# Gates and low parts in PSUM banks, GpSimd in pieces of 512 columns, the rounding of w_out on ScalarE: one change to a kernel of attention and two dense layers

## The chip, the cores and the metric

One core of a Trainium2 chip runs the whole program. The metric is the device time in microseconds. Of the kernel before there are three runs, median 811.41 us, from 811.0 to 811.67.

The engines are named as in the profile: PE is TensorE (PEld its weight load), DVE VectorE, ACT ScalarE, POOL GpSimd, SP SyncE, which issues nearly all loads and stores.

## The reference

```python
# attention: 2 x 8 heads, 768 tokens, 64 wide; mask: equal 6-bit sign buckets of q @ proj and k @ proj
scores = where(mask, (q @ k.T) / 8, -1e9)
attn = softmax(scores)            # sum + 1e-9
x = (attn @ v)                    # laid out as 1536 tokens x 512
# layer 1: 512 -> 2048 -> 512
h = x @ w_in;  g = where(h > 0, h, exp(min(h, 0)) - 1);  x = g @ w_out
# layer 2: 512 -> 2048 -> 512, its own weights
h = x @ w_in;  g = s * max(h, 0) ** 2 + b;  out = g @ w_out
```

All data are float32.

## The kernel before

Each float32 operand of a matrix product is held as two parts, "hi" (rounded to the short form that TensorE multiplies at full rate) and "lo" (the value less hi), and each product is three: hi x hi, hi x lo, lo x hi. Making hi is called rounding, making lo splitting.

**Attention.** Eight pairs of heads run one after the other, 12 units of 128 query rows to a pair. In each pair GpSimd splits q, k, v and every third transposed block (`split_third`), adds and scales the outputs into `x32` (`sum_x`, `scale_x`), and has slots for preparing the layers (`first_parts(i, half)`, two in a pair): it combines, rounds and splits the first weights, the first two blocks of w_out (`weights_out(0, 0)` and `(0, 1)`, the second in the slot (4, 0)) and the first chunk of x. SyncE asks for the second w_out block in pair 4 as well.

**The layers.** Each layer works on three chunks of 512 tokens (`CHUNKS`; q counts chunks through both layers, 0 to 5) and, for a chunk, in 8 steps of 256 hidden features (p = 0 to 7): 24 steps a layer (`LAYER`), 48 in all. A step has three parts.

1. `hidden(step)`, TensorE: the 512-deep product for 256 features x 512 tokens is done with seven block products instead of eight (`PRODUCTS`), from sums and differences of the blocks of w and x. Seven products of 6 matmuls with 256 columns (42 matmuls) go to four PSUM banks `h_ps[0..3]`, in the order of banks 0, 1, 2, 3, 0, 1, 3. Product 5 (bank 0 again) waits for ScalarE's copy of product 1 to `p1_sb` (shown as p_sb), product 6 (bank 1) for VectorE's sum U2, product 7 (bank 3) for U3. Products 1 to 4 wait for the sums C11, C12, C22, C21 of the step before.
2. The gate. VectorE makes the seven sums U2, U4, U3, C22, C11, C12, C21 (`sums`), each of one bank and one SBUF tile; the C sums are the hidden values, in `h_sb[0]` and `h_sb[1]`. For each half f ScalarE makes relu(-h) and exp(-that) (second layer: relu(h) and its square) in `r_sb[f]`; VectorE makes the gate in place in `h_sb[f]` (lines 1276 and 1278); ScalarE rounds it to `g_hi` (line 978 is the helper `copy` for all its copies); VectorE makes `g_lo` (line 1283). All of these are in SBUF.
3. `output(step)`, TensorE: 24 matmuls of 512 columns into the four banks `acc`, summed over the 8 steps of a chunk.

TensorE's order is hidden(step), output(step - 1), hidden(step + 1), and so on, so gates have the time of an output to be made. Its order at the start is: products 1 to 4 of hidden(0), the last pair's last P.V products, products 5 to 7, hidden(1), output(0).

VectorE's queue for a step: the sums, two gates, two low parts, `combine_w(step + 2)` (four additions of 256 columns, both operands in SBUF, which make the weight blocks' sums `wi_sum`), at p = 2 and 3 two operations each of `combine_x` for the next chunk, and in the second layer at p = 0 `keep_out`, the copy of the four `acc` banks to SBUF. ScalarE's: p_sb, `round_w(step + 1)` (three copies, the last of 1024 columns), relu and exp of both halves, two g_hi, at p = 0 in the first layer the copies of `acc` to `x32`, at p = 3 to 6 one `round_x`. GpSimd's: `weights(step + 1)`, the split of 512, 256 and 1024 columns (lines 590 and 593), then in 14 steps `weights_out` (step 0 to 5: the first layer's blocks 2 to 7; step 18 to 25: the second layer's blocks), a rounding (line 609) and a split (line 611) of 1024 columns each, then at p = 3 to 6 one `split_x` of 512 or 1024 columns. hidden(step) waits for `w_split`, at p = 0 for all four splits of x as well.

SyncE runs one queue in order: `load_w(step + 3)` waits for the split of step + 1, `load_wo` (line 385) for the split of the block before, as there is one buffer `wo_raw`; then stores.

Of the kernel before, what the change touches and what calls it, by code (L numbers as in the profile page):

```python
# [21 lines left out]
GROUPS = UNITS // HT  # L22
# [88 lines left out]
def build(nc, qk, v, planes_in, ident_in_d, w1_in, w1_out, w2_in, w2_out, s2, b2, out, inv_d):  # L111
    ctx = ExitStack()
    with ctx:
# [191 lines left out]
        out_kept = sem("out_kept")  # L305
        end_kept = sem("end_kept")
# [14 lines left out]
        def _(sp):  # L321
# [190 lines left out]
        def _(pool):  # L512
# [131 lines left out]
            def split_x(c, n):  # L644

                hi, lo = xb_hi[c % 2], xb_lo[c % 2]
                if n == B11:
                    x, dst = first_tokens(c % CHUNKS, lo)
                    return nc.gpsimd.tensor_tensor(dst, x, first_tokens(0, hi)[1].bitcast(F32), ALU.subtract)
# [3 lines left out]
                return nc.gpsimd.tensor_tensor(flat(lo[:, n:n + 2]), flat(xb_sum[c % 2][:, n:n + 2]),  # L653
                                               flat(hi[:, n:n + 2]).bitcast(F32), ALU.subtract)

            def first_parts(i, half):
# [14 lines left out]
                elif (i, half) == (4, 0):  # L671
                    weights_out(0, 1)
# [70 lines left out]
            for step in range(2 * LAYER):  # L743
# [11 lines left out]
                if q + 1 < 2 * CHUNKS and 3 <= p < 7:  # L755
                    n = p - 3
# [5 lines left out]
        def _(pe):  # L762
# [213 lines left out]
        def _(act):  # L976
# [95 lines left out]
            round_w(1)  # L1072
            for step in range(2 * LAYER):
# [4 lines left out]
                if 2 <= step + 1 < 2 * LAYER:  # L1078
                    round_w(step + 1)
                for f in range(2):  # L1080
                    act.wait_ge(added, SUMS * step + (C21 if f else C12))
                    wait(act, g_made, 2 * step - 1 + f)
                    nc.scalar.activation(r_sb[f][:], h_sb[f][:], ACT.Relu, scale=1.0 if layer else -1.0).then_inc(r_done, 1)  # L1083
                    act.wait_ge(r_done, 2 * step + f + 1)
                    nc.scalar.activation(r_sb[f][:], r_sb[f][:], ACT.Square if layer else ACT.Exp,  # L1085
                                         scale=1.0 if layer else -1.0).then_inc(e_done, 1)
                for f in range(2):
                    act.wait_ge(g_made, 2 * step + f + 1)
                    wait(act, g_free, 2 * step + f + 1 - GRING)
                    copy(g_hi[(2 * step + f) % GRING][:], h_sb[f][:]).then_inc(g_hi_done, 1)  # L1090
                if p == 0 and 0 < q <= CHUNKS:

                    for n in range(KT):
# [4 lines left out]
                        cols = slice(n * TOKENS + (q - 1) * CHUNK, n * TOKENS + q * CHUNK)  # L1098
                        copy(x32[:, cols], acc[n][:]).then_inc(y_kept, 1)
# [5 lines left out]
            act.wait_ge(out_kept, KT * CHUNKS)  # L1105
# [4 lines left out]
        def _(dve):  # L1110
# [105 lines left out]
            def combine_x(q, later):  # L1216

                c, n = q % CHUNKS, 4 * (q - 1)
                to = [as_x(xb_sum[q % 2][:, m]) for m in range(4)]
                b11, b12, b21, b22 = [x_of(c, d, t) for d in range(2) for t in range(2)]  # L1220
                if not later:
# [6 lines left out]
                    tt(to[T1], b12, b11, ALU.subtract).then_inc(xb_combined, 1)  # L1228
                    tt(to[T3], b22, b12, ALU.subtract).then_inc(xb_combined, 1)
                else:  # L1230
                    dve.wait_ge(xb_combined, n + 2)
                    tt(to[T2], b22, to[T1], ALU.subtract).then_inc(xb_combined, 1)
                    dve.wait_ge(xb_combined, n + 3)
                    tt(to[T4], b21, to[T2], ALU.subtract).then_inc(xb_combined, 1)

            def sums(step, part):
# [5 lines left out]
                for n in part:  # L1242
# [27 lines left out]
            def gate(step):  # L1270
                layer = step // LAYER
                for f in range(2):
                    h, e = h_sb[f][:], r_sb[f][:]
                    dve.wait_ge(e_done, 2 * step + f + 1)
                    if layer == 0:
# [71 lines left out]
```

## Time and profile before

| | us |
|---|---|
| median of three runs | 811.41 |
| the profiled execution | 812.05 |
| its span | 810.2 |
| PE busy | 755.5 |
| DVE busy | 667.2 |
| POOL busy | 523.0 |
| ACT busy | 490.6 |
| mean granted TensorE clock, share of full | 0.972 |

The profile is of one execution. The span runs from its first instruction to its last; the execution's own time is 1.85 us more. Busy time of an engine includes the time in which a started instruction is held back. Matmuls are pipelined and overlap in the records, so PE at 93% is not at its peak. The granted clock is the share of 2.4 GHz that TensorE was given; it has two levels, 1.00 and 0.50 (1.2 GHz), and slices of the page show a mean. A row with x2 merges two instructions of a kind. Square brackets hold the idle time of the engine before the instruction and what ended it.

### The profile page before, as it was taken

To read this page: it belongs to the slowest core of one execution; us is meant where nothing else is said; L and a number is where in the kernel's file an instruction comes from. 1 tells how busy PE (TensorE), PEld (TensorE's weight loads), DVE (VectorE), ACT (ScalarE), POOL (GpSimd) and SP (SyncE) were. 2 spreads that over 40 slices of the span, in tenths; PEclk is the share of its full clock that TensorE was granted. 3 is DMA by queue.
4 is the path that set the end of the run, shared out by engine and by line. 5 is a ranking of instruction groups with operands and counts; after the bars stand their busy time and mean duration, and the time that the engine had idled before them with its cause. 6 is when DMAs were issued, how large, how long until landed. Compare 5 with 4: busy or idle time off the path is not lost.

```text
span 810.2 us, 13830 instructions
## 1 busy us (share of the span) xinstructions
PE 755.5 (93%) x4617; PEld 684.1 (84%) x4617; DVE 667.2 (82%) x1191; ACT 490.6 (61%) x919; POOL 523.0 (65%) x370
## 2 busy tenths in 40 slices
PE   8999999799997887999989989698999999999998
PEld 6999999799986776998879878687887899798997
DVE  6888888688879888888888889888888878887774
ACT  8888887688854435565656454355556555565551
POOL 6688997999987777444654568775465444644440
PEclk9999999899998998999999989899999999999999
DMA  6576557456223221111111212212110311113101
GB/s 172 141 185 175 147 124 176 111 124 167 68 76 105 72 84 53 53 53 53 29 50 53 79 52 78 78 57 75 52 53 27 109 48 53 53 53 105 52 1 53
DMA packets 78286, 67.81 MB, mean 84 GB/s; under 512 B 9284, under 2 KB 66964, under 8 KB 78228
## 3 DMA queue, kind: packets, MB, share of 16 engines
q1 hardware_dynamic: 77940, 66.80, 30.2%
q8 instruction: 33, 0.54, 0.3%
q10 hardware_dynamic: 288, 0.26, 0.1%
q14 instruction: 25, 0.20, 0.1%
HBM read 46.23 MB, written 3.19 MB: 61 GB/s over the span
## 4 chain that ended last, share of the span: by engine, by line
PE 49%; DVE 32%; ACT 9%; issue 5%; POOL 4%; DMA 1%; SPq 0%; DVEq 0%; POOLq 0%; ACTq 0%
PE acc L886 14%; PE h_ps L866 14%; DVE g_lo L1283 8%; PE pt_ps L814 6%; DVE h_sb L1276 6%; ACT r_sb L1083 3%; PE pv_ps L829 3%; PE pv_ps L830 3%; PE s_ps L801 3%; PE s_ps L800 3%; DVE wi_sum L1212 3%; DVE h_sb L1278 3%; DVE wi_sum L1209 3%; ACT r_sb L1085 2%; DVE u_sb L1247 1%
## 5 line engine op out<-in xcount | busy, mean ns | idle before, releaser
L866 PE MATMUL h_ps<-xb_hi,wi_hi 128*128 128x256 f32 x672 | 198.6, 296 | 43.6 <-DVE u_sb L1247 36.8
L590 POOL TENSOR_TENSOR wi_lo<-w_raw,wi_hi 128x512 fp32r<-128x512 f32 x96 | 95.5, 1017 | 185.9 <-ACT wi_hi L978 185.9
L866 PE MATMUL h_ps<-xb_hi,wi_lo 128*128 128x256 f32 x672 | 193.4, 288 | 0.0
L866 PE MATMUL h_ps<-xb_lo,wi_hi 128*128 128x256 f32 x672 | 193.4, 288 | 0.0
L866 PEld LDWEIGHTS h_ps<-xb_hi,wi_hi 128*128 128x128 f32 x672 | 131.2, 195 | 53.3 <-DVE u_sb L1247 41.3
L866 PEld LDWEIGHTS h_ps<-xb_lo,wi_hi 128*128 128x128 f32 x672 | 131.8, 196 | 1.8
L866 PEld LDWEIGHTS h_ps<-xb_hi,wi_lo 128*128 128x128 f32 x672 | 131.9, 196 | 0.0
L593 POOL TENSOR_TENSOR wi_lo<-wi_sum,wi_hi 128x1024 fp32r<-128x1024 f32 x48 | 124.2, 2588 | 0.0
L1283 DVE TENSOR_TENSOR g_lo<-h_sb,g_hi 128x512 fp32r<-128x512 f32 x96 | 100.6, 1071 | 4.6 <-ACT g_hi L978 2.4
L1126 DVE TENSOR_SCALAR_CACHE_REDUCE probs<-s_ps 128x768 f32<-128x768 f32 x96 | 91.8, 957 | 11.1 <-PE s_ps L801 8.6
L978 ACT ACTIVATE g_hi<-h_sb 128x512 fp32r<-128x512 f32 x96 | 59.0, 626 | 67.4 <-DVE h_sb L1276 44.7
L886 PE MATMUL acc<-g_hi,wo_late 128*128 128x512 f32 x288 | 97.0, 409 | 0.0
L1276 DVE SCALAR_TENSOR_TENSOR h_sb<-r_sb,h_sb 128x512 f32<-128x512 f32 x48 | 79.3, 1666 | 21.2 <-ACT r_sb L1085 20.8
L978 ACT ACTIVATE wi_hi<-w_raw 128x512 fp32r<-128x512 f32 x94 | 44.0, 516 | 85.4 <-DVE wi_sum L1214 85.4
L886 PE MATMUL acc<-wo_late,g_hi 128*128 128x512 f32 x288 | 91.7, 390 | 0.0
L1083 ACT ACTIVATE r_sb<-h_sb 128x512 f32<-128x512 f32 x96 | 60.0, 625 | 52.0 <-DVE h_sb L1264 52.0
L984 ACT ACTIVATE probs<-probs,row_min 128x768 f32<-128x768 f32 x96 | 90.0, 937 | 2.1 <-DVE probs L1126 1.3
L814 PE MATMUL pt_ps<-ident_sb,probs 128*128 128x128 f32 x576 | 81.6, 278 | 5.8 <-ACT pt_raw L978 4.1
L814 PEld LDWEIGHTS pt_ps<-ident_sb,probs 128*128 128x128 f32 x576 | 69.1, 143 | 12.8 <-ACT pt_raw L978 4.4
L1278 DVE TENSOR_SCALAR h_sb<-r_sb,sb_scale 128x512 f32<-128x512 f32 x48 | 53.0, 1120 | 28.6 <-ACT r_sb L1085 28.6
L829 PE MATMUL pv_ps<-pt_hi,v_nat 128*128 128x384 f32 x192 | 72.8, 379 | 0.1
L886 PEld LDWEIGHTS acc<-g_hi,wo_late 128*128 128x128 f32 x288 | 58.2, 202 | 12.2
(116 smaller groups left out, 1747.7 us busy)
## 6 DMA issues: line engine op xcount, KB each, us to landing
w_raw<-w_in_dram SPq DMA_DIRECT2D x96, 256.0 KB, 3.1
wo_raw<-w_out_dram SPq DMA_DIRECT2D x32, 256.0 KB, 2.9
raw<-qk_dram SPq DMA_DIRECT2D x15, 384.0 KB, 5.4
qqk<-kt SPq DMA_DIRECT2D x15, 384.0 KB, 4.0
raw_v<-v_dram SPq DMA_DIRECT2D x16, 192.0 KB, 4.2
all_inv<-inv_dram SPq DMA_DIRECT2D x16, 192.0 KB
x_parts<-x_second SPq DMA_DIRECT2D x16, 192.0 KB, 5.4
qqk<-qqk SPq DMA_DIRECT2D x15, 192.0 KB, 2.7
```

The source lines that it names most:

```text
L590: nc.gpsimd.tensor_tensor(flat(lo[:, j]), loaded[:, cols], flat(hi[:, j]).bitcast(F32), ALU.subtract)
L593: return nc.gpsimd.tensor_tensor(flat(wi_lo[buf][:, S1:A11]), flat(wi_sum[buf][:]), flat(wi_hi[buf][:, S1:A11]).bitcast(F32), ALU.subtract)
L814: last = nc.tensor.transpose(pt_ps[n][:, r * P:(r + 1) * P], probs[k % SRING][:, (n * HT + r) * P:(n * HT + r + 1) * P], ident_sb[:])
L829: mm(pv_ps[:, 0:HALF], v_nat[par][:, kt, :], pt_hi[buf][:, kt, :], start=kt == 0, stop=False)
L866: last = mm(h_ps[bank][:, 0:Q], w[i][:, k * P:(k + 1) * P], x[j][:, k * Q:(k + 1) * Q], start=k == 0 and m == 0, stop=k == DK - 1 and m == 2)
L886: last = mm(acc[n][:], lhs, rhs, start=p == 0 and f == 0 and j == 0, stop=p == STEPS - 1 and f == 1 and j == 2)
L978: return nc.scalar.activation(dst, src, ACT.Copy)
L984: nc.scalar.activation(scores[:], scores[:], ACT.Exp, bias=row_min[:, k:k + 1], scale=-1.0, accum_out=row_sum[:, k, 0:1]).then_inc(exp_don ...
L1083: nc.scalar.activation(r_sb[f][:], h_sb[f][:], ACT.Relu, scale=1.0 if layer else -1.0).then_inc(r_done, 1)
L1126: ts(probs[k % SRING][:].rearrange("p (n c) -> p n c", n=2), s_ps[k % 2][:, :, 0:HALF], -SCALE, CEILING, ALU.mult, ALU.min, accum_out=row_ ...
L1276: last = nc.vector.scalar_tensor_tensor(h, e, 1.0, h, ALU.subtract, ALU.max)
L1283: tt(g_lo[n][:], h_sb[f][:], g_hi[n][:].bitcast(F32), ALU.subtract).then_inc(g_ready, 1)
```

## The change

- The exponential (the square) goes to bank `h_ps[f]`, the gate to bank `h_ps[2 + f]`; `g_hi` and `g_lo` are made from that bank. Products 1 and 2 of the next step wait for the two gates, products 3 and 4 for the two low parts, in place of the C sums.
- GpSimd's operations of 1024 columns on the weights' sums, on w_out's low part and on x are made in two of 512.
- ScalarE rounds w_out's blocks from the third on (`round_wo`, ahead of relu in its queue); GpSimd only splits them.
- In the attention, `weights_out(0, 1)` moves from the slot (4, 0) to (5, 0), and the combining and rounding of the first x move around it.
- hidden(0) is one piece ahead of the last P.V products; VectorE's `keep_x(PAIRS, -1)` moves behind all seven sums; ScalarE's `round_w(1)` moves behind the first p_sb.
- `combine_x` makes one difference a step at p = 1 to 4 instead of two at p = 2 and 3; `split_x` is at p = 4 to 7 instead of 3 to 6, behind weights and w_out.
- ScalarE copies `acc` of the first two chunks of the second layer too; VectorE copies the last chunk's (`keep_last`).

```diff
@@ SyncE, store(c)
-                        sp.wait_ge(out_kept, tile + 1)
+                        if c < CHUNKS - 1:
+                            sp.wait_ge(out_kept, tile + 1)
+                        else:
+                            sp.wait_ge(last_kept, m + 1)
@@ GpSimd
             def split_sums(buf):
-                return nc.gpsimd.tensor_tensor(flat(wi_lo[buf][:, S1:A11]), flat(wi_sum[buf][:]),
-                                               flat(wi_hi[buf][:, S1:A11]).bitcast(F32), ALU.subtract)
+                for j in (slice(S1, S3), slice(S3, A11)):
+                    last = nc.gpsimd.tensor_tensor(flat(wi_lo[buf][:, j]), flat(wi_sum[buf][:, j]),
+                                                   flat(wi_hi[buf][:, j]).bitcast(F32), ALU.subtract)
+                return last
...
                 pool.wait_ge(wo_landed, 32 * n + 32)
-                if layer:
-                    pool.wait_ge(g_free, 2 * (LAYER - STEPS + step) + 2)
-                nc.gpsimd.tensor_copy(wo(step, 0), wo_raw[:]).then_inc(wo_hi_done, 1)
+                if n < EARLY:
+                    nc.gpsimd.tensor_copy(wo(step, 0), wo_raw[:]).then_inc(wo_hi_done, 1)
                 pool.wait_ge(wo_hi_done, n + 1)
-                nc.gpsimd.tensor_tensor(wo(step, 1), wo_raw[:], wo(step, 0).bitcast(F32), ALU.subtract).then_inc(wo_split, 1)
+                for cols in (slice(0, DM), slice(DM, W)):
+                    last = nc.gpsimd.tensor_tensor(wo(step, 1)[:, cols], wo_raw[:, cols], wo(step, 0)[:, cols].bitcast(F32),
+                                                   ALU.subtract)
+                last.then_inc(wo_split, 1)
...
                 elif (i, half) == (4, 0):
+                    combine_x0(T1)
+                elif (i, half) == (4, 1):
+                    pool.wait_ge(x_scaled, PAIRS)
+                    combine_x0(T3, T2)
+                elif (i, half) == (5, 0):
                     weights_out(0, 1)
-                elif (i, half) == (4, 1):
-                    pool.wait_ge(x_scaled, PAIRS)
-                    combine_x0(T1, T3)
-                elif (i, half) == (5, 0):
-                    combine_x0(T2, T4)
                 elif (i, half) == (5, 1):
-                    round_x0(B11, B22)
+                    combine_x0(T4)
+                    round_x0(B11)
                 elif (i, half) == (6, 0):
+                    round_x0(B22)
                     round_x0(T1)
...
-                if step == 0:
-                    pool.wait_ge(pv_done, GROUPS * PAIRS)
...
-                if q + 1 < 2 * CHUNKS and 3 <= p < 7:
-                    n = p - 3
+                if q + 1 < 2 * CHUNKS and p >= 4:
+                    n = p - 4
@@ TensorE, hidden(step), the waits ahead of products 0 to 3
-                        wait(pe, added, SUMS * (step - 1) + C11)
+                        wait(pe, g_made, 2 * step - 1)
                     elif n == 1:
-                        wait(pe, added, SUMS * (step - 1) + C12)
+                        wait(pe, g_made, 2 * step)
                     elif n == 2:
-                        wait(pe, added, SUMS * (step - 1) + C22)
+                        wait(pe, g_ready, 2 * step - 1)
                     elif n == 3:
-                        wait(pe, added, SUMS * (step - 1) + C21)
+                        wait(pe, g_ready, 2 * step)
...
-            hidden(0, range(4))
+            hidden(0)
             times_v(PAIRS, -1, range(TILES))
-            hidden(0, range(4, NP))
@@ ScalarE
-            round_w(1)
+            def round_wo(layer, step):
+                n = layer * STEPS + step
+                act.wait_ge(wo_landed, 32 * n + 32)
+                if layer:
+                    act.wait_ge(g_free, 2 * (LAYER - STEPS + step) + 2)
+                copy(wo(step, 0), wo_raw[:]).then_inc(wo_hi_done, 1)
             for step in range(2 * LAYER):
...
                 copy(p1_sb[step % 2][:], h_ps[0][:, 0:Q]).then_inc(p1_kept, 1)
-                if 2 <= step + 1 < 2 * LAYER:
+                if step + 1 < 2 * LAYER:
                     round_w(step + 1)
+                if EARLY <= step + EARLY < STEPS:
+                    if step == 0:
+                        act.wait_ge(pv_done, GROUPS * PAIRS)
+                    round_wo(0, step + EARLY)
+                elif 0 <= step - (LAYER - STEPS + 2) < STEPS:
+                    round_wo(1, step - (LAYER - STEPS + 2))
...
-                    nc.scalar.activation(r_sb[f][:], r_sb[f][:], ACT.Square if layer else ACT.Exp,
+                    nc.scalar.activation(h_ps[f][:], r_sb[f][:], ACT.Square if layer else ACT.Exp,
...
-                    copy(g_hi[(2 * step + f) % GRING][:], h_sb[f][:]).then_inc(g_hi_done, 1)
-                if p == 0 and 0 < q <= CHUNKS:
+                    copy(g_hi[(2 * step + f) % GRING][:], h_ps[2 + f][:]).then_inc(g_hi_done, 1)
+                if p == 0 and q > 0:
...
+                        if q <= CHUNKS:
...
+                        else:
+                            wait(act, out_stored[n], 16 * (q - CHUNKS - 1))
+                            copy(o_sb[n], acc[n][:]).then_inc(out_kept, 1)
...
-                    act.wait_ge(xb_combined, 4 * q + 4 if n == 3 else 4 * q + 3)
+                    act.wait_ge(xb_combined, 4 * q + (1, 1, 3, 4)[n])
@@ VectorE
-            def gate(step):
...
+            def gate(step, f):
+                h, e, g = h_sb[f][:], h_ps[f][:], h_ps[2 + f][:]
+                dve.wait_ge(e_done, 2 * step + f + 1)
+                dve.wait_ge(added, SUMS * step + C21)
+                if step < LAYER:
+                    last = nc.vector.scalar_tensor_tensor(g, e, 1.0, h, ALU.subtract, ALU.max)
+                else:
+                    last = ts(g, e, sb_scale[:, 0:1], sb_scale[:, 1:2], ALU.mult, ALU.add)
+                last.then_inc(g_made, 1)
+            def gate_lo(step, f):
+                n = (2 * step + f) % GRING
+                dve.wait_ge(g_hi_done, 2 * step + f + 1)
+                tt(g_lo[n][:], h_ps[2 + f][:], g_hi[n][:].bitcast(F32), ALU.subtract).then_inc(g_ready, 1)
...
-            sums(0, (U2, U4, U3, C22))
+            sums(0, (U2, U4, U3, C22, C11, C12, C21))
             keep_x(PAIRS, -1)
-            sums(0, (C11, C12, C21))
...
-                if q + 1 < 2 * CHUNKS and 2 <= p < 4:
-                    combine_x(q + 1, p == 3)
-                if p == 0 and q > CHUNKS:
-                    keep_out(q - CHUNKS - 1)
-            keep_out(CHUNKS - 1)
+                if q + 1 < 2 * CHUNKS and 1 <= p < 5:
+                    combine_x(q + 1, (T1, T3, T2, T4)[p - 1])
+            keep_last()
```

## Rows read from the trace of the kernel before

**Rows 1.** The profile page: busy time with share and count; granted clock, 40 slices, tenths.
```profile
PE 755.5 (93%) x4617; PEld 684.1 (84%) x4617; DVE 667.2 (82%) x1191; ACT 490.6 (61%) x919; POOL 523.0 (65%) x370
...
PEclk9999999899998998999999989899999999999999
```
**Rows 2.** Stretches of the layers: us, busy time (instructions), granted clock, DMA share, GB/s.
```profile
339.70:381.00 41.30, 41.30 (x262) 37.53 (x261) 35.48 (x63) 25.41 (x45) 17.39 (x12) 1.00 0.19 54
455.00:534.00 79.00, 66.50 (x355) 58.35 (x355) 69.99 (x84) 35.73 (x60) 59.29 (x34) 0.89 0.23 70
509.46:516.29 6.83, 5.54 (x19) 4.96 (x20) 5.05 (x12) 4.91 (x8) 3.93 (x3) 0.50 0.01 2
```
**Rows 3.** Waits, 300 us to the end: total us, times, longest us.
```profile
PE h_ps L866 <- DVE u_sb L1247: 29.5, 18, 4.3
```
**Rows 4.** Timeline of ScalarE, the p_sb copy of four steps: start us, us, instruction.
```profile
258.83 0.38 ACT L978 ACTIVATE p_sb<-h_ps 128x256 f32<-128x256 f32 x1 [2.19 <-PE h_ps L866]
...
749.65 0.38 ACT L978 ACTIVATE p_sb<-h_ps 128x256 f32<-128x256 f32 x1 [2.44 <-PE h_ps L866]
...
760.15 0.38 ACT L978 ACTIVATE p_sb<-h_ps 128x256 f32<-128x256 f32 x1 [2.44 <-PE h_ps L866]
...
791.65 0.38 ACT L978 ACTIVATE p_sb<-h_ps 128x256 f32<-128x256 f32 x1 [2.44 <-PE h_ps L866]
```
**Rows 5.** Instructions by line, VectorE: ns min/median/max, first and last start, form.
```profile
L1276 DVE SCALAR_TENSOR_TENSOR h_sb<-r_sb,h_sb x48: 677/1569/2917, 240.6 to 532.4; 128x512 f32<-128x512 f32 x48
...
L1283 DVE TENSOR_TENSOR g_lo<-h_sb,g_hi x96: 677/693/2892, 243.3 to 799.5; 128x512 fp32r<-128x512 f32 x96
...
L1278 DVE TENSOR_SCALAR h_sb<-r_sb,sb_scale x48: 534/599/2469, 542.5 to 798.2; 128x512 f32<-128x512 f32 x48
...
L1247 DVE TENSOR_TENSOR u_sb<-h_ps,p_sb x48: 410/418/428, 236.3 to 792.4; 128x256 f32<-128x256 f32 x48
```
**Rows 6.** Timeline of one undisturbed step, all engines (TensorE left out).
```profile
353.27 1.04 ACT L978 ACTIVATE wi_hi<-wi_sum 128x1024 fp32r<-128x1024 f32 x1
...
355.19 0.63 ACT L1083 ACTIVATE r_sb<-h_sb 128x512 f32<-128x512 f32 x1 [0.87 <-DVE h_sb L1264]
355.45 0.42 DVE L1267 TENSOR_TENSOR h_sb<-h_ps,u_sb 128x256 f32<-128x256 f32 x1 [0.29 <-PE h_ps L866]
...
356.34 2.40 POOL L593 TENSOR_TENSOR wi_lo<-wi_sum,wi_hi 128x1024 fp32r<-128x1024 f32 x1
...
356.52 3.38 DVE L1276 SCALAR_TENSOR_TENSOR h_sb<-r_sb,h_sb 128x512 f32<-128x512 f32 x2 [0.64 <-ACT r_sb L1085]
...
361.63 0.38 ACT L978 ACTIVATE p_sb<-h_ps 128x256 f32<-128x256 f32 x1 [1.07 <-PE h_ps L866]
```
**Rows 7.** Timeline in the attention: GpSimd's second w_out block, VectorE's first x_parts of three pairs.
```profile
137.57 1.04 POOL L609 CAST wo_early<-wo_raw 128x1024 fp32r<-128x1024 f32 x1 [4.34 <-DMA wo_raw<-w_out_dram]
...
134.96 0.56 DVE L1154 COPY x_parts<-pv_ps 128x384 f32<-128x384 f32 x1 [0.37 <-PE pv_ps L830]
...
168.68 0.56 DVE L1154 COPY x_parts<-pv_ps 128x384 f32<-128x384 f32 x1 [0.36 <-PE pv_ps L830]
...
195.69 0.56 DVE L1154 COPY x_parts<-pv_ps 128x384 f32<-128x384 f32 x1 [0.36 <-PE pv_ps L830]
```
**Rows 8.** Timeline of VectorE, end of step 0 and start of step 1's sums.
```profile
245.96 1.31 DVE L1212 TENSOR_TENSOR wi_sum<-wi_sum,w_raw 128x256 f32<-128x256 f32 x1
247.30 1.14 DVE L1214 TENSOR_TENSOR wi_sum<-w_raw,wi_sum 128x256 f32<-128x256 f32 x1
248.36 0.41 DVE L1247 TENSOR_TENSOR u_sb<-h_ps,p_sb 128x256 f32<-128x256 f32 x1
```
**Rows 9.** GpSimd's groups by form, us and mean ns; landing times of line 385.
```profile
L590 POOL TENSOR_TENSOR wi_lo<-w_raw,wi_hi 128x512 fp32r<-128x512 f32 x41 | 53.1, 1294 | 171.1 <-ACT wi_hi L978 171.1
L590 POOL TENSOR_TENSOR wi_lo<-w_raw,wi_hi 128x256 fp32r<-128x256 f32 x41 | 30.4, 741 | 0.0
...
DMA to landing us min/median/max: 2.6/2.9/9.6
```

More of the change, by code:

```diff
@@ L305, in build @@
         out_kept = sem("out_kept")
+        last_kept = sem("last_kept")
         end_kept = sem("end_kept")
@@ L648, in split_x @@
                     x, dst = first_tokens(c % CHUNKS, lo)
-                    return nc.gpsimd.tensor_tensor(dst, x, first_tokens(0, hi)[1].bitcast(F32), ALU.subtract)
+                    for k in (slice(0, DK), slice(DK, KT)):
+                        last = nc.gpsimd.tensor_tensor(dst[:, k], x[:, k], first_tokens(0, hi)[1][:, k].bitcast(F32), ALU.subtract)
+                    return last
                 if n == B22:
@@ L652, in split_x @@
                                                    ALU.subtract)
-                return nc.gpsimd.tensor_tensor(flat(lo[:, n:n + 2]), flat(xb_sum[c % 2][:, n:n + 2]),
-                                               flat(hi[:, n:n + 2]).bitcast(F32), ALU.subtract)
+                for j in (n, n + 1):
+                    last = nc.gpsimd.tensor_tensor(lo[:, j], xb_sum[c % 2][:, j], hi[:, j].bitcast(F32), ALU.subtract)
+                return last
             def first_parts(i, half):
@@ L1214, in combine_w, with combine_x @@
                 tt(to[S4], raw_w[1], to[S2], ALU.subtract).then_inc(w_combined, 1)
-            def combine_x(q, later):
-                c, n = q % CHUNKS, 4 * (q - 1)
+            def combine_x(q, n):
+                c, done = q % CHUNKS, 4 * (q - 1)
                 to = [as_x(xb_sum[q % 2][:, m]) for m in range(4)]
                 b11, b12, b21, b22 = [x_of(c, d, t) for d in range(2) for t in range(2)]
-                if not later:
+                if n == T1:
                     if q < CHUNKS:
@@ L1256, in sums @@
                         dve.wait_ge(added, done + U3)
-                        wait(dve, g_ready, 2 * step)
+                        wait(dve, g_made, 2 * step)
                         last = tt(h_sb[1][:, other], bank[2], u3, ALU.add)
@@ L1268, in sums, with keep_last @@
                     last.then_inc(added, 1)
-            def gate(step):
[L1271 to L1275, printed above, removed]
-                        last = nc.vector.scalar_tensor_tensor(h, e, 1.0, h, ALU.subtract, ALU.max)
-                    else:
-                        last = ts(h, e, sb_scale[:, 0:1], sb_scale[:, 1:2], ALU.mult, ALU.add)
-                    last.then_inc(g_made, 1)
-                for f in range(2):
-                    n = (2 * step + f) % GRING
-                    dve.wait_ge(g_hi_done, 2 * step + f + 1)
-                    tt(g_lo[n][:], h_sb[f][:], g_hi[n][:].bitcast(F32), ALU.subtract).then_inc(g_ready, 1)
-            def keep_out(c):
+            def gate(step, f):
[11 more added lines that the diff above has]
+                tt(g_lo[n][:], h_ps[2 + f][:], g_hi[n][:].bitcast(F32), ALU.subtract).then_inc(g_ready, 1)
+            def keep_last():
                 for n in range(KT):
                     if n < KT - 1:
-                        dve.wait_ge(acc_done, (CHUNKS + c) * (KT - 1) + n + 1)
+                        dve.wait_ge(acc_done, 2 * CHUNKS * (KT - 1) - KT + n + 2)
                     else:
-                        dve.wait_ge(g_free, 2 * (LAYER + c * STEPS + STEPS))
-                    wait(dve, out_stored[n], 16 * c)
-                    if c == CHUNKS - 1 and n == KT - 1:
+                        dve.wait_ge(g_free, 4 * LAYER)
+                    dve.wait_ge(out_stored[n], 16 * (CHUNKS - 1))
+                    if n == KT - 1:
                         nc.vector.tensor_copy(o_sb[n][:, 0:END], acc[n][:, 0:END]).then_inc(end_kept, 1)
@@ L1296, in keep_out @@
                         last = nc.vector.tensor_copy(o_sb[n], acc[n][:])
-                    last.then_inc(out_kept, 1)
+                    last.then_inc(last_kept, 1)
             keep_x(PAIRS, -2)
@@ L1313, in _ @@
                     sums(step, (U2, U4, U3, C22, C11, C12, C21))
-                gate(step)
+                for f in range(2):
+                    gate(step, f)
+                for f in range(2):
+                    gate_lo(step, f)
                 if step + 2 < 2 * LAYER:
                     combine_w(step + 2)
-                if q + 1 < 2 * CHUNKS and 2 <= p < 4:
-                    combine_x(q + 1, p == 3)
-                if p == 0 and q > CHUNKS:
-                    keep_out(q - CHUNKS - 1)
-            keep_out(CHUNKS - 1)
+                if q + 1 < 2 * CHUNKS and 1 <= p < 5:
+                    combine_x(q + 1, (T1, T3, T2, T4)[p - 1])
+            keep_last()
 def x_cols(i, n):
```

28 lines of the change are left out of this document (16 added, 12 removed).

## The prediction

> **What bounds the kernel now.** I read the page first, then the stretches, then who waits for whom, then single instructions. The page [rows 1] shows TensorE busy for 93% of the span, but its granted clock falls below full speed around slices 7, 12 to 16 and 23 to 26, so something stops it there. The stretches of the two layers [rows 2] say where: from 339.7 to 381 us TensorE is busy all the time at full clock; from 455 to 534 us it is busy for 66.5 of 79 us at 0.89, and inside it 6.83 us from 509.46 run at 0.50. The waits of the layers [rows 3] name the releaser: TensorE stands 29.5 us for VectorE's U2 (the sum that frees bank 1 for product 6). GpSimd's long waits for ScalarE cost nothing by themselves.
>
> The size comes from ScalarE's copy of product 1 (p_sb), once a step. Step 2's starts at 258.83, step 47's at 791.65: 532.8 us for 45 steps. In undisturbed steps it comes every 10.50 us (749.65 and 760.15 are neighbours) [rows 4]. 45 x 10.50 = 472.5, so 60.3 us are lost to idle and to the half clock (1.2 GHz) after it.
>
> Why is U2 late? VectorE's gate takes 677 ns at best, 1569 in the median and 2917 at worst; the low part 677 to 2892; but U2, with one operand in a bank and one in SBUF, 410 to 428 in all 48 steps [rows 5]. The undisturbed step shows the mechanism [rows 6]: GpSimd's 1024-column operation runs from 356.34 for 2.40 us, and the first gate, started at 356.52, ends only after it (two gates take 3.38 us instead of twice 0.68), while the sums around them keep their 0.42 us whatever GpSimd does. An operation with both operands in SBUF waits for GpSimd's running one to end; one that reads a bank does not. The Trainium skill, "SBUF — State Buffer", section "Who interferes with whom", says the same (at most one SBUF input does not contend, two do, for the whole instruction). By that rule, the trace agrees, and nothing below needs it.
>
> **The change, part by part.**
>
> *Attention, -6.7 us.* GpSimd stands 4.34 us, until 137.57, for the load of the second w_out block, and the splits queued behind it come late. The pair in which that falls takes 33.72 us (134.96 to 168.68), the next 27.01 (to 195.69) [rows 7]. The change puts a 1.29 us combination in that place and the split one half pair later, with some 10 us more for the load. What moves in (one operation more in the next places, at most 1.3 us, as some slots before carried 3.4 without a stall) I cost at nothing; the cover is GpSimd's own spare time, and if it is gone a pair loses up to 1.3. Bounds -7 and 0. I take -6.7.
>
> *Hidden(0) in one piece, and the first steps, +0.5.* All seven products now come before the last P.V products. Hidden(1) waits for weights(1) as before, and now also for the gate of step 0, which ScalarE starts only after pv_done and a 1.05 us rounding of w_out. U2(1), at 248.36 before [rows 8], has no held gates ahead of it and comes some 2 us sooner. But step 1's rounding, and relu behind it, wait for w_out block 3. Its load is asked for after GpSimd's last x (the one that VectorE's 245.96 operation waits out, to 247.0, and 1.1 later now, as keep_x stands behind all seven sums) and the low part of block 2 (2.6 us): 250.7; with some 4 us to land (my estimate, between the usual 2.9 plus 0.5 for the issue and the longest 9.6, [rows 9]), 1.05 of rounding and 1.9 for relu, exp and gate, step 2 starts near 258, where it did. Bounds -3 and +4, I take +0.5.
>
> *Gates and low parts in banks, smaller pieces: the 60.3 us.* Let P be the start of a step's p_sb copy. The copy at 361.63 [rows 6] puts P of that step at 351.13 (10.50 earlier): C21 at P+4.3; relu, exp, relu, exp from P+4.06, 0.63 each; gates, no longer held, end at P+6.1 and P+7.35; low parts at P+8.0 and P+8.8; combine_w (4 x 0.34) follows to P+10.2; U2 may start as late as P+12.8 without TensorE noticing. New waits: product 1 of the next step comes at P+9.6 and needs the first gate (3.5 us to spare), product 4 at P+11.75 and needs the second low part (2.95 to spare). So a step is held by TensorE alone: -60.3, unless pieces of GpSimd still get in the way (next part). Second-layer gates: 534 ns at best now with one SBUF operand, against 677 for two [rows 5]. The Trainium skill, "VectorE: DVE Perf Modes", section "Why PSUM operands drop a tier", says that fp32 from a bank loses the double rate. By the rows this is at most 0.15 us a gate, 0.3 a step, inside the 2.95; by the rule some 0.3 us a gate, inside it too.
>
> *ScalarE rounds w_out.* 1.05 us more for it in 14 steps, 1.5 less for GpSimd. ScalarE's queue is p_sb, weights (to about P+2.3), w_out (1.04 us for 1024 columns [rows 6], to P+3.3), and relu wants to start at P+4.06. GpSimd runs P+2.35 to P+6.8 (1.29 for 512 columns, 0.74 for 256 [rows 9], and two more of 1.25), the w_out pieces to P+9.3; the next load lands 2.9 us after the last issue [rows 9], 0.5 later, at about the next P+2.2. It fits with 0.8 us to spare: nothing.
>
> *What comes back.* combine_w has both operands in SBUF, and the operations at 245.96 and 247.30 (1.31 and 1.14 us, where 0.42 is usual) each sit out one GpSimd operation of some 1.25 us when these come back to back [rows 8]. Two pieces (w_out or x alone): the first operation waits to P+9.3 and U2 is in time. Four pieces (both; layer 1, steps 4 and 5; the last four steps of the third chunk): they end at P+9.3, 10.55 and 11.8, combine_w at P+12.5; the rounding of the next weights starts some 1.7 us late, and with it GpSimd and relu; U2 misses by 2.0 and 0.4 us in the first chunk, by 0.8 and 2.4 in the third. At a chunk's end the last x split must be done at P+9.6. With weights and two pieces it ends at P+9.3: just in time, 1.0 after the first chunk and 1 for the other three. At the end of the third chunk the w_out pieces stand ahead of it: 4.1 us. That is long enough for the half clock: TensorE's longest idle before, 4.3 us [rows 3], lies in the slow stretch, and 6.83 us at 0.50 [rows 2] lose 3.4. Sum: 2.0+0.4+1.0+1.0+0.8+2.4+4.1+3.4 = 15.1 us. Bounds 3 and 35.
>
> *ScalarE keeps the second layer's outputs*, 4 x 0.6 us in three steps, in the idle time before p_sb, as in the first layer (TensorE is busy throughout the first stretch of [rows 2], which holds such a step). The end is VectorE's as before. Nothing, bounds 0 and 2.
>
> Sum against the profiled execution's 812.05 us: -6.7 + 0.5 - 60.3 + 15.1 = -51.4, 760.65. The runs' median is 0.64 lower than that execution (811.41): 760.0 us.
>
> **Rivals.**
> *Nothing comes back*: pieces and operations fall between each other as in the second layer's quiet steps. 760.0 - 15.1 = 745. For it: the x split alone fits. Against: both kinds in one step are 7 pieces of GpSimd in 10.5 us.
> *The w_out ring is the bound*: load, ScalarE, GpSimd, load is now a loop over three engines with 0.8 us to spare; a landing or a piece some 2 us late (late ones reach 9.6 us, [rows 9]) delays relu, then combine_w, then the next weights. At 1.6 us in each of 14 steps it adds 22: 782. For it: one buffer. Against: landings of 2.6 to 2.9 are the rule.
> *Slower: banks don't free the gates.* A gate that writes a bank and reads one might still be held, for no row shows an operation of VectorE that writes a bank. Then the long waits stay (up to 2.2 us for each of two gates and a low part, 6.7 a step), and TensorE, which before needed only the sums, waits for them in products 1 to 4. It decides where they pass the spare 2.95: by up to 3.7 us in 14 steps, a third of that on average, 17 us, on top of what is lost now: 811.4 - 6.7 + 17 = 822. Against it: the sums and the attention's reads from banks never waited.
> *The attention's stall stays* in another place (block 2 lands late again): 767.
>
> **Chances.** Forecast (752 to 772) 0.55, nothing back 0.17, ring 0.15, attention's stall 0.06, banks don't free the gates 0.05, no change 0.02. Under 0.2% either way could not be told from no change. Range: from the second case's 745 to the ring's 782, with a little for its bounds, 746 to 785. Faster 0.93, same 0.02, slower 0.05.
>
> **What would show it.** Gates near 0.7 us in every step and low parts too; p_sb 10.50 us apart except in steps 4 to 8 and 20 to 24; TensorE's longest idle ahead of step 24, released by GpSimd's xb_lo; no wait of GpSimd for wo_raw in the attention, pairs of 27 us; most of the half clock gone. It is wrong if gates exceed 1 us, if relu waits behind the w_out rounding in most steps, or if TensorE waits for g_made or g_ready beyond the first two steps.

## The result and the profile after

The changed kernel takes 759.4 us (median of 4 runs, 759.28 to 759.58) against 811.2 for the kernel before: ratio 0.9363, 95% interval 0.9347 to 0.9379. The forecast was 760.0. The profiled execution of the changed kernel has a span of 757.4 us.

The page answers to [rows 1]: TensorE's clock is at nine tenths or more in all 40 slices (mean 0.993, before 0.972), VectorE is busy for 92 us less, and the chain that ended last is TensorE's for 79%.

```profile
PE 735.4 (97%) x4617; PEld 670.9 (89%) x4617; DVE 574.7 (76%) x1183; ACT 503.0 (66%) x941; POOL 500.2 (66%) x438
...
PEclk9999999999999999999999999999999999999999
...
PE 79%; POOL 7%; issue 5%; DVE 4%; ACT 3%; DMA 2%; SPq 0%; POOLq 0%; DVEq 0%; ACTq 0%
```

Four stretches, columns as in [rows 2]: two in which TensorE never stops, one of them 231 us long, and two of half clock, one in step 2 and one after the idle at the end of the third chunk.

```profile
252.97:256.20 3.23, 3.23 (x17) 3.23 (x17) 3.09 (x8) 1.28 (x4) 0.00 (x0) 0.50 0.46 156
...
340.00:403.00 63.00, 63.00 (x398) 57.24 (x397) 45.45 (x94) 37.32 (x64) 35.80 (x31) 1.00 0.17 51
...
495.31:498.72 3.41, 3.41 (x19) 3.41 (x18) 0.42 (x1) 2.56 (x5) 0.33 (x1) 0.50 0.00 0
507.00:738.00 231.00, 231.00 (x1454) 209.91 (x1453) 165.97 (x336) 137.28 (x239) 119.12 (x104) 1.00 0.19 57
```

ScalarE's p_sb copies, as [rows 4]: 10.50 us apart in a quiet stretch, and 486.05 us from step 2's to step 47's, 13.6 more than 45 x 10.50, where it was 60.3.

```profile
252.79 0.38 ACT L989 ACTIVATE p_sb<-h_ps 128x256 f32<-128x256 f32 x1
...
707.34 0.38 ACT L989 ACTIVATE p_sb<-h_ps 128x256 f32<-128x256 f32 x1 [2.50 <-PE h_ps L878]
...
717.84 0.38 ACT L989 ACTIVATE p_sb<-h_ps 128x256 f32<-128x256 f32 x1 [2.50 <-PE h_ps L878]
...
738.84 0.38 ACT L989 ACTIVATE p_sb<-h_ps 128x256 f32<-128x256 f32 x1 [2.50 <-PE h_ps L878]
```

VectorE by line (ns min/median/max), as [rows 5]: minimum and maximum of each gate and of the low part are now within 13 ns. No gate and no low part is held.

```profile
L1308 DVE SCALAR_TENSOR_TENSOR h_ps<-h_ps,h_sb x48: 698/700/700, 235.6 to 488.0; 128x512 f32<-128x512 f32 x48
...
L1310 DVE TENSOR_SCALAR h_ps<-h_ps,sb_scale x48: 817/818/818, 502.7 to 745.4; 128x512 f32<-128x512 f32 x48
...
L1316 DVE TENSOR_TENSOR g_lo<-h_ps,g_hi x96: 679/686/692, 237.2 to 746.9; 128x512 fp32r<-128x512 f32 x96
```

In the attention, as [rows 7]: the pair that took 33.72 us takes 27.06, the next 27.20, and GpSimd splits the second w_out block at 160.91, and neither its rounding (at 159.77) nor the split has a wait ahead of it.

```profile
135.03 0.56 DVE L1184 COPY x_parts<-pv_ps 128x384 f32<-128x384 f32 x1 [0.37 <-PE pv_ps L841]
...
162.09 0.56 DVE L1184 COPY x_parts<-pv_ps 128x384 f32<-128x384 f32 x1 [0.37 <-PE pv_ps L841]
...
189.29 0.56 DVE L1184 COPY x_parts<-pv_ps 128x384 f32<-128x384 f32 x1 [0.36 <-PE pv_ps L841]
...
160.91 2.53 POOL L617 TENSOR_TENSOR wo_early<-wo_raw,wo_early 128x512 fp32r<-128x512 f32 x2
```

What TensorE still waits for from 225 us on (total, times, longest), against [rows 3]:

```profile
PE h_ps L878 <- DVE h_ps L1308: 6.1, 2, 3.3
PE h_ps L878 <- issue: 5.7, 2, 4.4
PE h_ps L878 <- DVE u_sb L1280: 2.9, 3, 1.4
```

The first row is the new wait for gates, ahead of steps 1 and 2 (3.33 and 2.77 us). The second, ahead of steps 8 and 24, has no releaser by name; the timeline gives it. TensorE's row is step 24's first matmul, after 4.38 us of idle; GpSimd's queue ahead of it, for step 23, is weights (484.80 to 489.3), w_out (to 492.0) and the last split of x, which ends at 494.77, 0.1 us before TensorE starts.

```profile
484.80 2.00 POOL L594 TENSOR_TENSOR wi_lo<-w_raw,wi_hi 128x512 fp32r<-128x512 f32 x2 [2.28 <-ACT wi_hi L989]
486.75 2.56 POOL L599 TENSOR_TENSOR wi_lo<-wi_sum,wi_hi 128x512 fp32r<-128x512 f32 x2
489.26 2.71 POOL L617 TENSOR_TENSOR wo_late<-wo_raw,wo_late 128x512 fp32r<-128x512 f32 x2
491.93 2.84 POOL L665 TENSOR_TENSOR xb_lo<-xb_sum,xb_hi 128x512 fp32r<-128x512 f32 x2
...
494.87 0.36 PE L878 MATMUL h_ps<-xb_hi,wi_hi 128*128 128x256 f32 x1 [4.38 <-issue]
```

### The profile page after: what moved, and what is told of

Same layout as the page of the kernel before. It is cut to its first block, busy times and chain, and to the rows that moved or that the text cites. A ratio compares the mean times of both kernels' runs of the same rounds, so it can differ in the third digit from the quotient of the medians.

```text
span 757.4 us, 14021 instructions
## 1 busy us (share of the span) xinstructions
PE 735.4 (97%) x4617; PEld 670.9 (89%) x4617; DVE 574.7 (76%) x1183; ACT 503.0 (66%) x941; POOL 500.2 (66%) x438
## 4 chain that ended last, share of the span: by engine, by line
PE 79%; POOL 7%; issue 5%; DVE 4%; ACT 3%; DMA 2%; SPq 0%; POOLq 0%; DVEq 0%; ACTq 0%
PE acc L898 31%; PE h_ps L878 29%; PE pt_ps L825 6%; PE pv_ps L841 3%; PE pv_ps L840 3%; PE s_ps L812 3%; PE s_ps L811 3%; POOL pt_lo L532 1%; POOL pt_hi L530 1%; POOL x L548 1%; DMA all_inv<-inv_dram 1%; ACT r_sb L1108 1%; DVE wi_sum L1242 1%; DVE wi_sum L1240 1%; POOL x_sum L539 1%
## 5 line engine op out<-in xcount | busy, mean ns | idle before, releaser
L878 PE MATMUL h_ps<-xb_hi,wi_hi 128*128 128x256 f32 x672 | 193.6, 288 | 14.8 <-DVE h_ps L1308 6.1
L599 POOL TENSOR_TENSOR wi_lo<-wi_sum,wi_hi 128x512 fp32r<-128x512 f32 x96 | 122.5, 1298 | 0.0
L898 PE MATMUL acc<-g_hi,wo_late 128*128 128x512 f32 x288 | 91.8, 390 | 0.0
L989 ACT ACTIVATE p_sb<-h_ps 128x256 f32<-128x256 f32 x48 | 18.4, 383 | 92.0 <-PE h_ps L878 91.4
L1316 DVE TENSOR_TENSOR g_lo<-h_ps,g_hi 128x512 fp32r<-128x512 f32 x96 | 65.8, 685 | 3.6
L1163 DVE TENSOR_TENSOR pt_lo<-pt_ps,pt_hi 128x384 fp32r<-128x384 f32 x128 | 65.1, 550 | 2.0 <-ACT pt_hi L989 1.9
L989 ACT ACTIVATE g_hi<-h_ps 128x512 fp32r<-128x512 f32 x96 | 56.7, 590 | 14.8 <-DVE h_ps L1310 8.8
L811 PE MATMUL s_ps<-kt,qqk 128*128 128x384 f32 x192 | 65.6, 342 | 0.3 <-DVE probs L1156 0.3
L989 ACT ACTIVATE pt_hi<-pt_ps 128x384 fp32r<-128x384 f32 x128 | 55.9, 489 | 14.6 <-PE pt_ps L825 14.5
```

The lines of the kernel that those rows point to most:

```text
L599: last = nc.gpsimd.tensor_tensor(flat(wi_lo[buf][:, j]), flat(wi_sum[buf][:, j]), flat(wi_hi[buf][:, j]).bitcast(F32), ALU.subtract)
L811: mm(s_ps[buf][:, n, 0:HALF], q1, kt1[ops][:, cols], start=True, stop=False)
L878: last = mm(h_ps[bank][:, 0:Q], w[i][:, k * P:(k + 1) * P], x[j][:, k * Q:(k + 1) * Q], start=k == 0 and m == 0, stop=k == DK - 1 and m == 2)
L898: last = mm(acc[n][:], lhs, rhs, start=p == 0 and f == 0 and j == 0, stop=p == STEPS - 1 and f == 1 and j == 2)
L989: return nc.scalar.activation(dst, src, ACT.Copy)
L1316: tt(g_lo[n][:], h_ps[2 + f][:], g_hi[n][:].bitcast(F32), ALU.subtract).then_inc(g_ready, 1)
```

## Experiments

Two kernels (e_banks, e_waits) start from the kernel before, all others from the changed one. Times are medians with their range, ratios are to the kernel before, run beside it, and differences in us are of medians. The edits are shown in part; "..." marks what is left out.

**e_sbuf: the gates back in SBUF.**

```diff
-                        wait(pe, g_made, 2 * step - 1)
+                        wait(pe, added, SUMS * (step - 1) + C11)
...
-                h, e, g = h_sb[f][:], h_ps[f][:], h_ps[2 + f][:]
+                h, e, g = h_sb[f][:], r_sb[f][:], h_sb[f][:]
...
```

> The changed kernel with gates, exponentials and low parts back in SBUF and TensorE's waits back on the C sums; all else (pieces of 512, w_out rounded by ScalarE, the order) stays. My theory, that the banks free VectorE from GpSimd: the gates and low parts wait again, for at most 1.3 us each instead of 2.9, so gates show medians above 0.9 us and the time is 775 to 800 us. Rival, that the smaller pieces did the work and the banks are ornament: 757 to 765 us.

803.6 us (802.0 to 806.5), ratio 0.9901 (0.9870 to 0.9931): 44.2 us of the gain are gone. Its gate has a median of 1296 ns and a maximum of 1784, between [rows 5] and after, as pieces of half the size would give. It lost more than the 775 to 800 us that I expected: the two rows of waits show U2 again, and 15.4 us with no named releaser, all ahead of a chunk's first step (8, 16, 24, 32 and 40). GpSimd's rows ahead of step 8 say why: its two pieces of weights take 3.46 us and its two of x 3.37, against 2.55 and 2.70 in the changed kernel. The hold goes both ways: GpSimd's pieces are slowed by VectorE's too. x ends at 333.73, and step 8 starts at 333.84.

```profile
L1307 DVE SCALAR_TENSOR_TENSOR h_sb<-r_sb,h_sb x48: 691/1296/1784, 237.2 to 520.5; 128x512 f32<-128x512 f32 x48
...
PE h_ps L878 <- DVE u_sb L1280: 22.3, 14, 3.6
PE h_ps L878 <- issue: 15.4, 5, 3.8
...
326.94 3.46 POOL L599 TENSOR_TENSOR wi_lo<-wi_sum,wi_hi 128x512 fp32r<-128x512 f32 x2
330.36 3.37 POOL L665 TENSOR_TENSOR xb_lo<-xb_sum,xb_hi 128x512 fp32r<-128x512 f32 x2
```

**e_banks: the banks alone**, in the kernel before.

```diff
-                        wait(pe, added, SUMS * (step - 1) + C11)
+                        wait(pe, g_made, 2 * step - 1)
...
-                    h, e = h_sb[f][:], r_sb[f][:]
+                    h, e, g = h_sb[f][:], h_ps[f][:], h_ps[2 + f][:]
...
```

> The kernel before with the banks alone: exponentials, gates and low parts work on h_ps, TensorE waits for gates and low parts; pieces of 1024, GpSimd's rounding, the attention's slots and all else as before. Theory (the banks carry the gain, taking them away cost 44 us): 811.2 - 44 = 767 us (762 to 775), of which 5.8 are the attention's stall. Rival, that the banks are worth 44 us only beside the other edits: 780 us or more.

767.1 us (767.0 to 769.9), ratio 0.9458 (0.9438 to 0.9479): 44.1 us alone, 44.2 when taken away. The banks are the change's main part by both. That the two agree within 0.1 us is partly chance: e_sbuf's loss holds waits for x ahead of a chunk's first step (15.4 us against 5.7 with the banks), and in e_banks, where x is split a step earlier, TensorE has no such wait.

**e_1024: GpSimd in one piece again.**

```diff
-                for j in (slice(S1, S3), slice(S3, A11)):
+                for j in (slice(S1, A11),):
...
-                for cols in (slice(0, DM), slice(DM, W)):
+                for cols in (slice(0, W),):
...
```

> The changed kernel with GpSimd's operations in one piece of up to 1024 columns again; gates stay in banks. My theory: only combine_w and combine_x still meet GpSimd, and they come after the weights' splits (P+8.8 against P+6.8), so quiet steps stay at 10.50 us, the steps with w_out and x together keep their misses with one longer wait in place of two, and each pair of pieces saves its 0.2 us: 755 to 764 us. Rival, that the pieces carry the gain: above 780 us.

757.6 us (756.3 to 758.1), ratio 0.9328 (0.9312 to 0.9344), against 0.9363 (0.9347 to 0.9379) with the pieces: undoing the pieces gains 1.8 us. TensorE's longest wait ahead of step 24 is shorter too (3.6 against 4.4 us). Once the gates are in banks, smaller pieces cost more than they spare.

**e_slot: the second w_out block in its old slot.**

```diff
                 elif (i, half) == (4, 0):
-                    combine_x0(T1)
+                    weights_out(0, 1)
...
```

> The changed kernel with the second w_out block split in the attention's slot (4, 0) again, as before the change. My theory: GpSimd waits some 4.3 us for the load again, one pair takes 33.7 us instead of 27.05: 766 us (764.5 to 767.5). Rival, that other work in the attention (pieces of 512, other places) took the stall away: 759 to 760 us.

765.2 us (763.9 to 766.4), ratio 0.9432 (0.9415 to 0.9448): +5.8 us. GpSimd's wait for the load is back, 2.86 us here, and the pair takes 32.1 us (134.93 to 167.03).

```profile
136.37 1.04 POOL L614 CAST wo_early<-wo_raw 128x1024 fp32r<-128x1024 f32 x1 [2.86 <-DMA wo_raw<-w_out_dram]
...
134.93 0.56 DVE L1182 COPY x_parts<-pv_ps 128x384 f32<-128x384 f32 x1 [0.37 <-PE pv_ps L839]
...
167.03 0.56 DVE L1182 COPY x_parts<-pv_ps 128x384 f32<-128x384 f32 x1 [0.37 <-PE pv_ps L839]
```

**e_gp_rounds: GpSimd rounds w_out.**

```diff
-                if n < EARLY:
-                    nc.gpsimd.tensor_copy(wo(step, 0), wo_raw[:]).then_inc(wo_hi_done, 1)
+                if layer:
+                    pool.wait_ge(g_free, 2 * (LAYER - STEPS + step) + 2)
+                for cols in (slice(0, DM), slice(DM, W)):
+                    last = nc.gpsimd.tensor_copy(wo(step, 0)[:, cols], wo_raw[:, cols])
+                last.then_inc(wo_hi_done, 1)
...
```

> The changed kernel with GpSimd rounding the w_out blocks again, in two pieces, ScalarE none. My theory: some 1.3 us more of GpSimd in 14 steps are hidden where w_out is alone, show in the six steps with x and at the end of the third chunk (+8), and ScalarE no longer holds step 1's relu for the load (-2 to -3 at step 2): 762 to 768 us. Rival, that GpSimd's work is the bound in every w_out step: 14 x 1.3 more, 775 us or above.

765.4 us (763.6 to 766.3), ratio 0.9428 (0.9407 to 0.9449): ScalarE's rounding is worth 6.0 us. TensorE waits 5.6 us ahead of step 24, and steps 5 and 21 take 4.1 and 4.4 us more than 10.50 (1.3 and 0.9 in the changed kernel); quiet steps stay at 10.50, and so do steps 18 and 19, which have w_out alone. Not every w_out step pays, which was the rival.

**e_waits: the kernel before with TensorE's new waits only.**

```diff
...
-                        wait(pe, added, SUMS * (step - 1) + C21)
+                        wait(pe, g_ready, 2 * step)
...
```

> The kernel before with only TensorE's four waits of the change (gates for products 1 and 2, low parts for products 3 and 4), operands still in SBUF. It prices my slower rival. In the profile before, the second low part ends up to 2.9 us after product 4's start in 10 steps, 14 us in sum: 820 to 830 us if that is what the waits cost; 811 us if they are free whatever the gates take.

812.3 us (810.4 to 813.6), ratio 1.0007 (0.9991 to 1.0024): no difference, against the 14 us that I had added up. The waits do bite; they take the place of another. From 225 us on, e_waits has these waits of TensorE,

```profile
PE h_ps L866 <- DVE u_sb L1247: 19.4, 15, 2.3
PE h_ps L866 <- DVE g_lo L1283: 16.1, 15, 1.8
PE h_ps L866 <- ACT p_sb L978: 5.6, 4, 2.3
PE h_ps L866 <- DVE h_sb L1276: 3.1, 2, 2.9
```

and the kernel before these:

```profile
PE h_ps L866 <- DVE u_sb L1247: 36.8, 21, 4.3
PE h_ps L866 <- ACT p_sb L978: 5.5, 5, 1.8
PE h_ps L866 <- POOL wi_lo L593: 1.3, 1, 1.3
```

44.2 us against 43.6. The low part and U2 stand in one queue on VectorE; a TensorE that has waited for the first comes later to product 6 and finds less to wait for there. That is not the whole account. The longest stop falls from 4.3 to 2.9 us, and the granted clock is higher. The same stretch in the kernel before (0.89) and in e_waits (0.94):

```profile
455.00:535.00 80.00, 67.50 (x361) 59.20 (x361) 70.99 (x84) 36.35 (x60) 60.29 (x34) 0.89 0.24 73
...
455.00:535.00 80.00, 66.49 (x364) 57.88 (x363) 71.00 (x84) 36.38 (x60) 59.68 (x34) 0.94 0.23 72
```

Against that stand more stops (36 against 27), each of which costs more than its recorded idle (in the changed kernel step 21 has 0.50 us of it and comes 0.90 late). How much of the zero is waits replaced and how much the clock's is not shown.

**Four kernels on what comes back.** Their edits, with the end of each expectation tested in turn.

e_later moves the w_out blocks of the second layer:

```diff
+OUT_STEPS = (18, 19, 24, 25, 26, 27, 28, 29)
...
-                elif 0 <= step - (LAYER - STEPS + 2) < STEPS:
-                    weights_out(1, step - (LAYER - STEPS + 2))
+                elif step in OUT_STEPS:
+                    weights_out(1, OUT_STEPS.index(step))
...
```

> The changed kernel with blocks 2 to 7 of the second layer's w_out prepared in steps 24 to 29 instead of 20 to 25, so that none falls into a step with a split of x. Theory (four pieces in a step are what costs): the excess of steps 21 to 24 over 10.50 us (0.9, 0.3, 6.4, 1.6 = 9.1 us) goes: 750.3 us (749 to 752). Rival, that the end of a chunk costs it whatever w_out does: 757 us or more.

753.3 us (753.2 to 754.7), ratio 0.9281 (0.9257 to 0.9304), 3 us above the forecast. Steps 21 to 24 are at 10.50, as expected, but steps 28 and 29 have both kinds again, an oversight of mine in the list: TensorE waits once more for U2, in step 29, and at the end of that chunk (1.3 us).

```profile
544.32 0.39 PE L879 MATMUL h_ps<-xb_hi,wi_hi 128*128 128x256 f32 x1 [0.49 <-DVE u_sb L1281]
```

e_xfirst splits x ahead of the weights:

```diff
+                if q + 1 < 2 * CHUNKS and p >= 4:
+                    n = p - 4
+                    pool.wait_ge(xb_hi_done, 4 * q + n + 1)
+                    split_x(q + 1, (B11, B22, T1, T3)[n]).then_inc(xb_split, 1)
                 if 2 <= step + 1 < 2 * LAYER:
                     weights(step + 1)
...
```

> The changed kernel with GpSimd's split of x ahead of the weights' split in its queue, where it stood idle for ScalarE's rounding; w_out as changed. Theory (at a chunk's end TensorE waits for x, which stands last): the waits ahead of steps 8 and 24 go, about 1.4 and 5 us, while x now meets combine_w in steps without w_out too: 752 to 757 us. Rival, that only the sum of GpSimd's work in a step counts: 758 to 760 us.

756.4 us (756.1 to 757.4), ratio 0.9318 (0.9295 to 0.9341). The waits ahead of steps 8 and 24 are gone (no row without a releaser is left), and those for U2 grew from 2.9 to 6.5 us: x now meets combine_w.

```profile
PE h_ps L877 <- DVE u_sb L1279: 6.5, 8, 1.4
PE h_ps L877 <- DVE h_ps L1307: 6.0, 2, 3.3
```

e_head rounds w_out behind g_hi in steps 0 and 1:

```diff
...
+                if step < 2:
+                    if step == 0:
+                        act.wait_ge(pv_done, GROUPS * PAIRS)
+                    round_wo(0, step + EARLY)
```

> The changed kernel with ScalarE's rounding of w_out behind the g_hi copies in steps 0 and 1. Theory (relu stood behind a load in step 1, behind pv_done in step 0): TensorE's 2.8 us ahead of step 2 go, and some 1 of the 3.3 ahead of step 1: 755.4 us (754 to 757). Rival, that the start hangs on the weights' splits and loads: 759 us.

757.9 us (757.5 to 758.5), ratio 0.9333 (0.9310 to 0.9356): 1.5 us, not 4. The wait for the gates is gone, and behind it stands GpSimd's split of the weights, 4.5 us in two waits. The start hangs on both.

```profile
PE h_ps L878 <- POOL wi_lo L599: 4.5, 2, 2.3
```

e_all is these three together.

> All three edits together. If the excess of the layers (14.2 us from step 2 on) is w_out beside x and x at the end of the queue, and the start's 4 us are relu's place: 744 us (742 to 748). If one of them only shifts the wait: 749 us or more.

752.6 us (752.5 to 753.0), ratio 0.9268 (0.9246 to 0.9290), where 742 to 748 was expected: the rival's side. Moving x to the front kept U2 late in steps 4 to 6 and 28 to 30, where both kinds stand, and in step 20.

**e_order: neither overlap.** x goes between weights and w_out, w_out skips the steps where x has two pieces, but for one at a chunk's end, and the roundings of steps 0 and 1 stand as in e_head.

```diff
+OUT0_STEPS, OUT1_STEPS = (0, 1, 2, 3, 5, 7), (18, 19, 21, 24, 25, 26, 27, 29)
...
+                if q + 1 < 2 * CHUNKS and p >= 4:
+                    n = p - 4
+                    pool.wait_ge(xb_hi_done, 4 * q + n + 1)
+                    split_x(q + 1, (B11, B22, T1, T3)[n]).then_inc(xb_split, 1)
+                if step in OUT0_STEPS:
+                    weights_out(0, OUT0_STEPS.index(step) + EARLY)
...
```

> The changed kernel with x split between weights and w_out in GpSimd's queue, the w_out blocks in steps 0, 1, 2, 3, 5, 7 and 18, 19, 21, 24 to 27, 29 instead of 0 to 5 and 18 to 25 (loads asked for behind the split of the block before), and in steps 0 and 1 ScalarE's rounding of w_out behind g_hi. If w_out beside x in following steps and ahead of x at a chunk's end is the excess: 14.2 us shrink to 3 or less, the start gives 1.5: 746 us (744 to 749). If each step with both still costs 1 us or more: 750 us or more.

747.4 us (747.0 to 747.8), ratio 0.9217 (0.9197 to 0.9237), as expected. No wait for U2 is left.

**e_order_1024: the same in one piece each.**

```diff
-                for j in (slice(S1, S3), slice(S3, A11)):
+                for j in (slice(S1, A11),):
...
```

> The same as e_order with GpSimd's operations in one piece of 1024. If a piece's fixed 0.2 us is all that the size matters: 0.5 to 2 us faster than e_order. If one longer hold hurts combine_w more than two short ones: slower than e_order.

744.9 us (744.2 to 746.1), ratio 0.9189 (0.9167 to 0.9211), the fastest of all and 14.5 us below the changed kernel. The size of the pieces shows again, by 2.5 us (0.5 to 2 expected). TensorE's waits from 225 us on are 5.1 us in four:

```profile
PE h_ps L877 <- POOL wi_lo L600: 3.5, 2, 2.0
PE h_ps L877 <- DVE u_sb L1280: 1.6, 2, 0.9
```

## Why the prediction was right

- *The bound.* TensorE alone sets the step once U2 is in time: 10.50 us in 231 us without a stop. The 60.3 us were rightly sized by p_sb's distances, which hold idle and slow clock in one number. The clock is up to 17 us of the gain (my estimate: 0.028 of a span of 810.2 us before, 0.007 of 757.4 after).
- *The mechanism.* e_sbuf and e_banks show it from both sides, 44.2 and 44.1 us. Gates that write a bank are not held, which no row of before had shown. My rule (both operands in SBUF wait, one in a bank does not) leaves out the second layer's gate: it reads one tile, reads and writes SBUF, and was held as well, to 2469 ns [rows 5]. With both in banks it is free too (817 to 818 ns).
- *Attention, -6.7.* In the trace the pair is 6.66 us shorter; undone in the changed kernel it costs 5.8, as the load, asked for 0.3 us later than before (129.79 against 129.52), landed 1.2 us sooner.
- *The start, +0.5.* Step 2's p_sb is 6.04 us earlier (258.83 to 252.79), of which 6.7 are the attention: +0.6. The copy itself starts 0.7 us late there, behind g_hi in ScalarE's queue, so that by TensorE's first matmuls the start gives nothing away (257.91 to 251.22 is 6.69). The reason given holds: ScalarE stood 6.08 us for block 3 and began to round at 248.14, then TensorE waited 2.77 us for the gate.

```profile
248.14 1.06 ACT L989 ACTIVATE wo_late<-wo_raw 128x1024 fp32r<-128x1024 f32 x1 [6.08 <-DMA wo_raw<-w_out_dram]
...
251.22 0.35 PE L878 MATMUL h_ps<-xb_hi,wi_hi 128*128 128x256 f32 x1 [2.77 <-DVE h_ps L1308]
```

- *What comes back, 15.1.* 13.6 by p_sb. The parts are less even: by the distances of the steps' first matmuls, which sum to 14.2, the first chunk's misses are 1.3 and 0.3 (forecast 2.0 and 0.4), the third's 0.9 and 0.3 (0.8 and 2.4), its last step and end 7.9 (4.1 + 3.4; in it are 1.4 us of waiting for U2 in step 23, 4.4 of idle, and 3.41 us at 0.50, which lose 1.7), the first chunk's end 1.6 (1.0), and the ends of the others nothing (1.0). The forecast had no term for step 2, which takes 2.0 us more than 10.50: after the stop of 2.77 us ahead of it the clock is 0.50 from 252.97 to 256.20. So the near hit of this sum is partly luck: one term is missing and the third chunk's are too high. combine_w meets pieces as drawn:

```profile
466.52 0.63 DVE L1239 TENSOR_TENSOR wi_sum<-w_raw 128x256 f32<-128x256 f32 x1
467.07 1.51 DVE L1240 TENSOR_TENSOR wi_sum<-w_raw 128x256 f32<-128x256 f32 x1
468.51 1.52 DVE L1242 TENSOR_TENSOR wi_sum<-wi_sum,w_raw 128x256 f32<-128x256 f32 x1
```

- *ScalarE's rounding, "nothing".* Right as a cost to ScalarE; as a gain it is 6.0 us, which stood unnamed inside the 60.3. Likewise the pieces: I took them as part of the cure, and they cost 1.8.
- *Second-layer gates.* I put the loss at 0.15 us a gate; it is 0.28 (534 to 818 ns). The Trainium skill's section "Why PSUM operands drop a tier" ("VectorE: DVE Perf Modes") was nearer: by that rule some 0.3 us (the prediction's estimate), the trace agrees. It stayed inside the step's slack: the second layer's quiet steps are at 10.50.
- *Rivals.* The slower one's price was wrong by its own logic: e_waits costs nothing, where I added 17 us. With banks that didn't free the gates, the time would, as an estimate, have been near e_sbuf's 804, and not 822; no run shows it. The w_out ring shows in step 1, where ScalarE stood 6.08 us, but not as the bound: steps 3, 4 and 18 to 20, with a block each, are at 10.50. "Nothing comes back" (745) was false for this order of work, and e_order_1024 reaches it with another.

By p_sb the parts (-6.7 + 0.6 - 60.3 + 13.6) give -52.8, the difference of the two spans. The edits taken one by one (44.2 + 6.0 + 5.8 - 1.8) give 54.2 us against the measured 51.8. The remaining edits (x a step later, `keep_last`, hidden(0) in one piece) weren't tried alone, so whether they cost the 2.4 us or the parts overlap is open.

## What to carry to other kernels

Size a loss by the distance between two marks of the loop, less the steps at their undisturbed length, and then ask which single wait ends last. When an engine's instructions on SBUF are held by a neighbour's, move operands, not the neighbour: with an operand in a bank the hold was gone here (gates of 1569 ns in the median before, 700 after), and cutting the neighbour's work into pieces then only added their fixed cost (two of 512 columns 2.55 us, one of 1024 columns 2.40). And lateness against each wait must not be added up: waits in one loop on one queue can replace each other.

## What the runs showed that I had not expected

- Four new waits that made TensorE stand 19.2 us in themselves (16.1 + 3.1) changed the time by 0.07% (interval -0.09% to +0.24%).
- A tensor_scalar of 512 columns from bank to bank takes 818 ns, more than the 700 ns of the two-operand gate from a bank and SBUF; from SBUF to SBUF it takes 534 when nothing holds it.
- ScalarE's rounding of 512 columns takes 590 ns on average from a bank, against 626 before from SBUF.
- Two additions of 256 columns on VectorE that meet GpSimd's pieces take 1.5 us each instead of 0.42, and GpSimd's pieces there take 1.4 instead of 1.29: both sides pay.
